# The buffer between the second and the third stage of a Fourier filter, turned from rows per time group to 33 words per channel

## What is computed

```python
def _attn_ref(x, filt_r, filt_i):            # x: (2, 3008, 256)
    X = np.fft.rfft(x, axis=1)
    Y = X * (filt_r + 1j * filt_i)[None, :, :]
    return np.fft.irfft(Y, n=x.shape[1], axis=1)
...
def _moe_ref(x, w_in, w_out):                # 6016 x 256 -> 2048 -> 256
    h = x @ w_in
    g = np.where(h > 0.0, h, np.exp(np.minimum(h, 0.0)) - 1.0)
    return g @ w_out
...
def _moe2_ref(x, w_in, w_out):
    h = x @ w_in
    return (h * np.clip(h + 3.0, 0.0, 6.0) / 6.0) @ w_out
```

## Time and profile before

| | us |
|---|---|
| three executions, median | 1119.72 |
| lowest, highest | 1117.58, 1120.87 |
| the profiled execution, its own time | 1119.74 |
| its span, first to last instruction | 1117.9 |
| TensorE busy | 1106.2 |
| VectorE busy | 743.9 |
| ScalarE busy | 750.9 |
| GpSimd busy | 289.9 |

### The profile page before, as it was taken

How to read it: one execution, slowest core, us unless ns; L and a number is a source line. 1 busy time by engine, 2 the same in 40 slices (tenths; PEclk the granted TensorE clock), 3 DMA queues, 4 the chain that set the end, 5 groups by cost and what they waited for, 6 DMA issues and landing times.

```text
span 1117.9 us, 13357 instructions
## 1 busy us (share of the span) xinstructions
PE 1106.2 (99%) x4840; PEld 891.0 (80%) x4840; DVE 743.9 (67%) x912; ACT 750.9 (67%) x1113; POOL 289.9 (26%) x228
## 2 busy tenths in 40 slices
PE   8999999999999999999999999999999999999998
PEld 4666788888888888888888788888888888888886
DVE  6777466666667666666677866666666665666665
ACT  0222588888788888888899766665666566666654
POOL 3877402102102111111288821111120120120000
PEclk9999999999999999999999999999999999999999
DMA  9977300200200200200311200200101001100000
GB/s 251 278 254 240 114 1 1 74 1 1 74 1 0 74 1 1 74 1 1 112 38 57 93 1 1 74 1 25 50 1 37 37 1 37 38 1 1 38 1 37
DMA packets 31185, 59.30 MB, mean 53 GB/s; under 512 B 3600, under 2 KB 19856, under 8 KB 31120
## 3 DMA queue, kind: packets, MB, share of 16 engines
q1 hardware_dynamic: 24784, 48.10, 13.2%
q10 hardware_dynamic: 6336, 10.36, 2.7%
HBM read 39.94 MB, written 18.51 MB: 52 GB/s over the span
## 4 chain that ended last, share of the span: by engine, by line
PE 91%; ACT 4%; DVE 2%; issue 1%; DMA 1%; POOL 0%; ACTq 0%
PE ps L390 43%; PE ps L381 13%; PE ps L380 13%; PE ps L379 13%; PE ps L347 2%; PE ps L322 2%; PE ps L338 2%; PE ps L339 2%; PE ps L330 2%; DVE e L643 1%; ACT e L516 1%; DMA w_raw<-w_dev 1%; ACT e L518 1%; ACT w_hi L495 1%; DVE g_lo L657 1%
## 5 line engine op out<-in xcount | busy, mean ns | idle before, releaser
L657 DVE TENSOR_TENSOR g_lo<-e,g_hi 128x502 fp32r<-128x502 f32 (+1 forms) x288 | 277.9, 992 | 136.0 <-ACT g_hi L548 135.8
L381 PE MATMUL ps<-op_lo,w_hi 128*128 128x502 f32 x672 | 261.9, 390 | 0.0
L379 PE MATMUL ps<-op_hi,w_hi 128*128 128x502 f32 x672 | 261.8, 390 | 0.0
L380 PE MATMUL ps<-op_hi,w_lo 128*128 128x502 f32 x672 | 261.2, 389 | 0.0
L390 PE MATMUL ps<-g_hi,w_hi 128*128 128x502 f32 x768 | 236.3, 389 | 2.0 <-ACT ystage L487 2.0
L390 PE MATMUL ps<-g_lo,w_hi 128*128 128x502 f32 x768 | 237.3, 390 | 0.9 <-DVE g_lo L657 0.7
L390 PE MATMUL ps<-g_hi,w_lo 128*128 128x502 f32 x768 | 235.5, 387 | 0.0
L726 POOL TENSOR_TENSOR op_lo<-op_raw,op_hi 128x1004 fp32r<-128x1004 f32 (+1 forms) x48 | 100.4, 2091 | 490.5 <-ACT op_hi L503 490.5
L390 PEld LDWEIGHTS ps<-g_hi,w_hi 128*128 128x128 f32 x768 | 144.0, 188 | 31.8 <-ACT ystage L487 2.4
L390 PEld LDWEIGHTS ps<-g_lo,w_hi 128*128 128x128 f32 x768 | 143.7, 188 | 31.8 <-DVE g_lo L657 3.2
L390 PEld LDWEIGHTS ps<-g_hi,w_lo 128*128 128x128 f32 x768 | 144.5, 188 | 29.3
(11 more groups left out here) (53 smaller groups left out, 1149.6 us busy)
## 6 DMA issues: line engine op xcount, KB each, us to landing
f_ring<-f_dev SPq DMA_DIRECT2D x32, 384.0 KB, 4.6
op_raw<-y SPq DMA_DIRECT2D x36, 251.0 KB, 3.6
x_ring<-x_dev SPq DMA_DIRECT2D x32, 192.0 KB, 5.1
y<-ystage SPq DMA_DIRECT2D x12, 502.0 KB, 2.8
out_dev<-ystage SPq DMA_DIRECT2D x12, 502.0 KB, 2.8
y<-ystage ACTq DMA_DIRECT2D x24, 235.0 KB, 3.1
w_raw<-w_dev ACTq DMA_DIRECT2D x16, 256.0 KB, 4.7
w_raw<-w_dev SPq DMA_DIRECT2D x16, 256.0 KB, 3.0
```

The costliest lines, as they stand in the source:

```text
L379: pe.matmul(out, w_hi[p][:, cols], hi, start=start, stop=False, skip_group_check=True)
L380: pe.matmul(out, w_lo[p][:, cols], hi, start=False, stop=False, skip_group_check=True)
L381: pe.matmul(out, w_hi[p][:, cols], lo, start=False, stop=True, skip_group_check=True).then_inc(done, 1)
L657: return dve.tensor_tensor(g_lo[:, tiles, :], e[:, tiles, :], f32(g_hi[:, tiles, :]), ALU.subtract)
```

## The change

Each half of `back` becomes 128 channels x 33 words: the channel d is the outer index, j the inner one, and the 33rd word of each channel stays unused. `turn_r` then writes, for each of its 16 channels, one run of 32 adjacent words, where before each word went 128 words (512 bytes) behind the last. `part_i` reads its stationary operand, 128 channels of one j, with a step of 33 words (132 bytes), where before it read 128 adjacent words. The number of products, loads, transpositions and their shapes stay as they were.

The larger buffer (33,792 bytes a partition for 32,768) comes with three adjustments. Of the last matrix I1 only the 94 columns in use are loaded (`MCOL`). The tiles `g_hi`, `g_lo`, `e` and `h2` are placed ahead of the `op1` tiles in memory. And SyncE's load for stage 1 now waits until all 28 pieces are done (`i_done`), since its target lies over a part of `back` that is read until then. The first instructions of the kernel, a memset and three products on zeros, use another stretch of `back`.

```diff
+JP = J + 1
+MCOL = (len(MATS) - 1) * P + ICOL
...
-            mats = sbuf(fft, "mats", [P, len(MATS) * P])
+            mats = sbuf(fft, "mats", [P, MCOL])
...
-            back = sbuf(fft, "back", [P, 2, J, P])
+            back = sbuf(fft, "back", [P, 2, P, JP])
+        g_hi = sbuf(ctx, "g_hi", [P, 4, T], F32R)
+        g_lo = sbuf(ctx, "g_lo", [P, 4, T], F32R)
+        e = sbuf(ctx, "e", [P, 4, T])
+        h2 = sbuf(ctx, "h2", [P, 2, T])
         op_hi.append(sbuf(ctx, "op1_hi", [P, 7, T], F32R))
...
                 if s == 1:
-                    sp.wait_ge(p1_done, 1)
+                    sp.wait_ge(i_done, NPIECE)
...
-            sp.dma_start(mats[:, 2 * P:], mats_dev[:, 2 * P:]).then_inc(mat_loaded["back"], 16)
+            sp.dma_start(mats[:, 2 * P:], mats_dev[:, 2 * P:MCOL]).then_inc(mat_loaded["back"], 16)
...
-                    last = pe.matmul(ps_i(n)[:, j * ICOL:j * ICOL + ICOL], back[:, pos % 2, j0 + j, :],
+                    last = pe.matmul(ps_i(n)[:, j * ICOL:j * ICOL + ICOL], back[:, pos % 2, :, j0 + j],
                                      mat("I1")[:, 0:ICOL], start=True, stop=True)
...
-                dst = back[:, pos % 2, :, g * GD:g * GD + GD].rearrange("p j d -> p d j")
-                dve.transpose(dst, ps_r(i)).then_inc(back_ready, 1)
-
-            dve.memset(back[:, 0, 0:4, :], 0.0).then_inc(zeroed, 1)
+                dve.transpose(back[:, pos % 2, g * GD:g * GD + GD, 0:J], ps_r(i)).then_inc(back_ready, 1)
+
+            dve.memset(back[:, 0, 0:16, :], 0.0).then_inc(zeroed, 1)
```

More of the change, by code:

```diff
@@ L130, in build @@
         op_lo.append(sbuf(ctx, "op1_lo", [P, 7, T], F32R))
[L131 to L134, removed]
         ps = ctx.enter_context(nc.psum_tensor("ps", [P, 8, 512], F32))
@@ L141, in mat @@
             at = MATS.index(name) * P
-            return mats[:, at:at + P]
+            return mats[:, at:min(at + P, MCOL)]
         def ps_i(n):
@@ L351, in _ @@
             pe.wait_ge(zeroed, 1)
+            zeros = back[:, 0].rearrange("p d j -> p (d j)")
             for _ in range(3):
-                pe.matmul(ps[:, 0, :], back[:, 0, 0, :], back[:, 0, 0:4, :].rearrange("p j d -> p (j d)"),
-                          start=True, stop=True)
+                pe.matmul(ps[:, 0, :], zeros[:, 0:P], zeros[:, 0:4 * P], start=True, stop=True)
             pe.wait_ge(mat_loaded["A"], 16)
```

## The result

The changed kernel takes 1148.37 us (median of four executions, 1146.89 to 1148.90), the kernel before 1119.37 us in the same comparison: a ratio of 1.0254, with an interval of 1.0241 to 1.0266. It is 29.0 us slower; 1143.6 was forecast. In the profiled executions the spans are 1145.1 and 1117.9 us, 27.2 us apart. That 27.2 is what the two traces can explain; the profiled execution of the changed kernel is the lowest of its four.

The account below looks back on a forecast made before the run. The prediction took TensorE's weight load in part_i as the bound. 24.1 us for longer loads less 0.2 us at the last transposition, +23.9 us on 1119.74, gave 1143.6 us; 8-in-10 range 1118 to 1150.

Parts of the forecast that it names:

- The bound of part_i: In part_i, the weight load sets the pace: 0.109 us a matmul, 0.84 to 0.85 ns a column.
- Which loads count: In part_i, 225 of 256 loads lie on the path; 28 first loads and three of the last piece are covered.
- The price of a load: In part_i, the 132-byte step makes each load 107 ns longer, +24.1 us in all.
- a second tick for each column: Strided weight load in part_i takes twice 0.84 ns a column; total 1143.6 us, own range 1139 to 1147, chance 0.57.
- Other addresses. Nothing on the path: Smaller I1, larger first memset and moved addresses: nothing on the path, all under 0.1 us.
- The last transposition: In unit 0, the first piece's wait for the last turn_r goes, its transposition being 0.36 us shorter: -0.2 us.
- The first steps: PE's 2.0 us of waits for DVE in the first steps: nothing taken, with 2.0 us as the bound.
- The later load for stage 1: SP's load now waits for i_done, at the end of unit 0: cost zero, hidden by 28 us before ScalarE's cast.
- The free load: Rival: part_i's strided load costs nothing, pitch stays 0.109 us; 1119.5 us, chance 0.25.
- The small price: Rival: 30 to 40 ns a load in part_i, if part of the latency hides; about 1127 us, chance 0.04.
- the faster case: Rival: over 0.3% (3.4 us) faster through shorter turn_r waits with a free load; 1115.5 us if all went, chance 0.02.
- The heavy price: Rival: part_i's step costs more than twice 0.84 ns a column, a load 159 ns longer; 1156 us, chance 0.12.

Follow-up runs that it names:

- 64-column pieces: Last pieces of the kernel before with the stationary read's step changed from piece to piece; these load 64 channels, not 128; whole kernel 1136.5 us.
- shifted kernel before: The kernel before with 32 bytes of unused memory ahead of op1_hi and op1_lo and 32 behind them; 1122.17 us, 1.0025 of the kernel before.
- kernel with the adjacent read: The changed kernel with the last stage reading 128 adjacent words, so multiplying wrong values; 1121.18 us, 1.0012 of the kernel before.
- three variants that keep the strided read: The changed kernel with 32 unused bytes ahead of op1_hi (1146.11 us), with 96 (1146.53 us), or with 32 words per channel, not 33 (1146.12 us).

## Why the prediction was right, and where it was short

- **The bound of part_i: right.** The forecast rested on reading 1.09 us for ten matmuls as the weight load's pace and not the moving side's. The 64-column pieces show it: with half the columns, adjacent, a piece falls from 1.09 to 0.95 us, near the moving side's 0.8; with step 32 it is the load's again; and 47 moving columns for 94 change nothing. The pitch of 0.109 us that the forecast read is the mean of nine pitches of 0.112 and one of 0.08.
- **Which loads count: right.** 256 - 28 - 3 = 225. A full piece has nine slow pitches and one of 0.08 us, and the last piece only shortened ScalarE's wait, by 0.4 us.
- **The price of a load: too low, the term that was mis-sized.** The step said "a second tick for each column", 107 ns, from a row of DVE and an argument on ticks. A full piece takes 2.15 us for the forecast 2.05. Measured are 0.230 - 0.112 = 0.118 us, and 225 x 0.118 = 26.6 us, 2.5 more than the 24.1 of the sum. The pitch at other steps runs from 218 to 267 ns, so it is no whole tick. At 33 words a column takes 0.230 / 128 = 1.80 ns, between the twice 0.84 of the forecast and the 1073 / 512 = 2.1 of DVE's strided write taken as a whole. With this term the time, 1148.37, lies just above the range of its own that the prediction gave the second tick (1139 to 1147), and inside the one of 8 in 10 (1118 to 1150). What makes 12 and 24 words dearer than 16 and 32 stays open.
- **"Other addresses. Nothing on the path": wrong by 1.7 us.** The change moved op1_hi and op1_lo from a multiple of 128 bytes to 32 short of one. The kernel that moves them back shows it alone: 981.5 us for the layer phase. The one that moved the tiles of the kernel before agrees with it but moved g_hi and g_lo too. What TensorE does there is not settled.
- **The last transposition, -0.2 us: right.** The three parts of the stretch of 99.59 us add up: 26.9 for the pieces by their lengths (27.46 us before, 54.41 after), less 0.36 for the last piece, less 0.2, is 26.4.
- **The first steps: nothing taken, and nothing shown.** The first piece started 0.9 us earlier in the changed kernel, but this start differs between the profiled executions of all kernels, and the two kinds overlap: 35.0 to 36.7 us in the six with a short transposition, 35.9 to 38.7 in the four with a long one. The 38.7 is the shifted kernel before, whose granted clock from 24 to 40 us was 0.96.
- **The later load for stage 1: right.** It was issued at 159.05 us and ScalarE's cast of it came at 186.66, with no wait:

```profile
159.05 0.33 SPq L273 DMA_DIRECT2D op_raw<-y  x1
...
186.66 1.02 ACT L505 CAST op_hi<-op_raw 128x1004 fp32r<-128x1004 f32 x1
```

- **The sum.** 1119.7 + 26.6 - 0.2 + 1.7 - 0.9 gives 1146.9, the profiled execution's 1146.89. Its terms are read off this execution, so that they add up tests their completeness and not the forecast. The median is 1.5 us above that, within the spread of the kernel before (1117.6 to 1120.9); no trace shows where those 1.5 us lie.
- **The rivals.** The free load (0.25) is out; it would have been right for a step of two words. The small price and the faster case are out too. The heavy price, 268 ns, is out for 33 words but is what a step of 12 has (267). The Trainium skill, TensorE: Matmul & The Clock Gate, section LDWEIGHTS, gives a load's time by its columns alone, 107 ns for 128 of them. The traces agree at steps 1 and 2 (0.112 and 0.118 us) and not at 33 (0.230).

## What to carry to other kernels

A strided access costs the engine that makes it, so before a stride is moved from a write to a read, ask which of the two engines has idle time: here it went from VectorE, a quarter idle, to TensorE, which had none, and 11.4 us saved against 26.6 lost became 26.6 lost. If both sides matter, lay the words out in pairs, so that the writer has two adjacent words and the reader a step of two; that was enough for VectorE's write in full and for TensorE's weight load but for 6 ns in 118. And when a buffer grows, look at where everything behind it in memory has moved.

## What was new about the hardware

- TensorE's weight load of 32 bit words: 112 ns for 128 adjacent columns, 118 with a step of 8 bytes, 173 with 12, and 218 to 267 with 16 to 132 bytes, with no growth by distance. An odd first word changes nothing (1.14 us for a piece of step 2 from word 1 as from word 0).
- A transposition's write is as fast in runs of two words as in runs of 32: 718 and 717 ns, against 1073 with each word 512 bytes from the last.
- Tiles of seven moving operands of 502 words that begin 32 or 64 bytes off a multiple of 128: 0.027 to 0.030 us more per unit, 10.2 us, with no wait in the trace. Tiles on an odd multiple of 128 bytes were read in units as slow as that (71.53 us for seven), but no run moved them. The operands within a tile are 2008 bytes apart, so most of them are off such a multiple either way; why the tile's start matters stays open.
- Behind a wait of 2.0 us, in a phase otherwise full, TensorE's granted clock fell to the level of 1.2 GHz for some 3.4 us in some profiled executions and not in others: it did in the kernel with the adjacent read, not in the one before, whose wait is the same 2.0 us. The mean granted clock was 0.998 or less in 11 of 23 executions of the kernel before, and 0.999 or 1.000 in all 13 of the changed kernel and its three variants that keep the strided read, where this wait is 1.6 us. That the shorter wait is the reason is not shown.
